# A fused attention and two-layer MLP kernel: gated values written where the sums read them, new orders on all engines

## The chip, the cores and the metric

One core of one Trainium2 chip. The metric is the device time of one execution in microseconds (us). The kernel has five instruction streams, each with its own order: TensorE (PE; its weight loads are shown as PEld), VectorE (DVE), ScalarE (ACT), GpSimd (POOL) and SyncE (SP), which here issues every DMA. Streams meet only at semaphores. Times of rows are us from the start of the span of one profiled execution.

## The reference

Attention over 4 x 8 heads of 576 tokens (a mean-pooled softmax attention, repeated to full length, plus a local one) gives x of 2304 x 512. Then two layers, all in fp32:

```
gate = 1 / (1 + exp(-(x @ w_gate)));  val = x @ w_val        # w_gate, w_val: 512 x 1536
x = (gate * val) @ w_out                                     # 1536 x 512
h = x @ w_in                                                 # 512 x 2048
g = h * (1 / (1 + exp(-1.702 * h)))
out = g @ w_out                                              # 2048 x 512
```

## The kernel before

**Precision.** A product of two fp32 matrices is made of three matmuls in the format fp32r: every operand is split into a rounded part (hi, a CAST on ACT) and the rest (lo, a subtraction on DVE or POOL); hi*hi, hi*lo and lo*hi are added in PSUM.

**Strassen's scheme.** Every product of layers 1 and 2 into the hidden dimension is a block of 2 x 2 quarters made of seven products p1 to p7 instead of eight. A product is six matmuls of 128 x 384 (two halves of the depth, three matmuls each). It needs sums of quarters of the weights (S1 to S4, made once, stored in DRAM as `w_split` and fetched for each block) and of x (T1 to T4, made once for each pass over 768 tokens; there are three passes for each layer). A block has three PSUM banks: x gets p1, then p6, p7 and p4 on top; y gets p2; z gets p5 and p3. ACT copies x out three times (`snap_p1`, `snap_u2`, `snap_u3`, lines 1069 to 1084); p6 waits for the first copy, p7 for the second, p4 for the third. DVE adds the copies to the other banks (`c11` line 1585, `c22` line 1595, `c12` line 1599); the four quarters of a result are called 11, 21, 12 and 22. p3 waits for `c22`, since z is read by it.

**Groups and pairs.** A group is 256 columns of the hidden dimension. In layer 1 it has two blocks (gate and value: 14 products), in layer 2 one (7). Groups 0 to 5 (layer 1, first pass) are multiplied by w_out in the plain way (`from_one_to_one`, `second`). Groups 6 to 41 are taken in pairs, and the output product of a pair is in Strassen's form too: `second_pair` (lines 776 to 778), seven tiles of two column blocks, six matmuls each, so 14 steps of one product's length. There are six pairs of layer 1 (`pair_of_one`, c = 6 to 16) and twelve of layer 2 (`pair_of_two`, c = 18 to 38, and `last_pair`). For c, the second group of the pair is d = c + 1, and n = c + 2 opens the next pair. The stages of a pair: PE runs p4 and p3 of c's last block, the blocks of d, all but p4 and p3 of n's first block, then the 14 steps.

**What the output product needs.** From the gated values: hi (`hi11`, ..., line 1150) and lo (`low11`, ..., line 1608) of quarters 11, 21 and 22, and of four sums T1 = g12 - g11, T3 = g22 - g12, T2 = T3 + g11, T4 = g21 - T2 (`make_t1`, ... lines 1644 to 1665 on DVE, `hi_t` line 1167 on ACT, `low_t` line 1669 on DVE). Gated values lie in the PSUM banks, written in place by `gate` (DVE, layer 1) or `gelu` (ACT, line 1109). Since T1 and T3 overwrite banks, ACT copies 11, 21 and 12 to SBUF first (`save11`, `save21`, `save12`, lines 1131, 1138, 1144), into a free part of the buffer `g_f`. From w_out (c's pair of groups): SP's `load_pair` (line 390) loads two blocks of 512 KB into `raw`; ACT rounds (`v_a12`, `v_a11`, `v_a22` line 1028 from `raw`; `v_s1` to `v_s4` line 1035 from sums); POOL makes the four sums (`pair_sum`, line 2036) and seven lo parts (`pair_low`, line 2040) in `split_pair`. The sum VS3 is made last, when the sixth tile of the pair before has been read. `load_pair(c + 2)` waits for all seven lo parts of c.

**Other work.** Eight jobs (`job_a`, `job_s` on ACT, `job_sums`, `job_lows` on POOL) split the weights of layer 2 during layer 1. Before each pass T1 to T4 of x are made (`next_t2_sums`, `next_t1_t3_sums`, `next_t4_sums` on POOL, lines 2074 to 2133), rounded on ACT (line 999), and their lo parts made on POOL (line 2067).

**What sets the order.** Every stream's order is written out by hand: `pair_of_one`, `pair_of_two` and `last_pair` exist once for ACT and once for DVE, `step` and `head` for PE, the loops at the end of the sync and gpsimd blocks for the rest. Each engine does its list in order, so an instruction that waits holds all behind it.

## Time and profile before

| what | us |
|---|---|
| median of 3 runs (lowest, highest) | 1040.64 (1037.27, 1041.56) |
| the profiled execution | 1044.47 |
| its span | 1042.8 |
| PE busy in it | 915.2 |
| PEld, DVE, ACT, POOL busy | 871.8, 585.1, 528.3, 594.9 |

The rows further below are lines of the profile. A group row of instructions reads: line, engine, operation, output<-inputs, shapes, count | busy us, mean ns of one | idle time before them and what ended it. "X <- Y" in a list of waits means that X started when Y had ended. Matmuls overlap, so that a busy time of PE counts more than the time between starts: the starts of two matmuls are what to read.

### The profile page before, as it was taken

Reading aid. Unit: us, or ns where it says so; the run is one execution under the profiler, and the core shown is the slowest. Engines: PE = TensorE matmul, PEld = TensorE weight load, DVE = VectorE, ACT = ScalarE, POOL = GpSimd, SP = SyncE. Lnnn points to the kernel's source line nnn. Section 1 sums busy time; section 2 is a strip of 40 time slices with the busy share of each in tenths; the row PEclk is TensorE's granted clock in tenths of the full one; section 3 lists DMA queues with packets and bytes.
Section 4 is the critical chain, followed back from the end, with each engine's and each line's share of the span. In section 5 each row is a group of like instructions: output and inputs, shape, how many; then the busy total and the mean of one; then the engine's idle time right before and its main releaser. Section 6 shows DMA issues by size and latency. Waiting matters only on the chain.

```text
span 1042.8 us, 18514 instructions
## 1 busy us (share of the span) xinstructions
PE 915.2 (88%) x6638; PEld 871.8 (84%) x6638; DVE 585.1 (56%) x1128; ACT 528.3 (51%) x1191; POOL 594.9 (57%) x483
## 2 busy tenths in 40 slices
PE   9999999997969898799898788888788888798798
PEld 7787999997868898798898788878788878788787
DVE  6677454453545555375555466555466555465476
ACT  5787645543445354355444545534545534534552
POOL 5688898897167375727365653444663444631531
PEclk9999999998989999999999999898999988898899
DMA  8775566875465946284936245335236425236321
GB/s 319 246 215 199 207 221 244 331 295 180 152 233 170 353 122 222 77 303 154 361 116 211 70 133 162 91 112 161 70 133 222 125 78 162 66 120 190 108 72 61
DMA packets 74778, 184.27 MB, mean 177 GB/s; under 512 B 5568, under 2 KB 31168, under 8 KB 71872
## 3 DMA queue, kind: packets, MB, share of 16 engines
q1 hardware_dynamic: 74688, 183.10, 51.4%
q8 instruction: 53, 0.87, 0.4%
q14 instruction: 37, 0.30, 0.1%
HBM read 141.66 MB, written 41.42 MB: 176 GB/s over the span
## 4 chain that ended last, share of the span: by engine, by line
PE 52%; POOL 19%; issue 10%; ACT 8%; DMA 6%; DVE 4%; SPq 1%; ACTq 0%; DVEq 0%; POOLq 0%
POOL v L2040 7%; PE o_ps L776 5%; POOL v_f L2036 5%; PE o_ps L778 5%; PE o_ps L777 5%; PE d_ps L632 4%; POOL xs_lo L2067 4%; DMA raw<-in_w_out_dram 4%; PE d_ps L633 4%; PE d_ps L634 4%; PE o_ps L623 4%; PE s_ps L632 3%; PE s_ps L634 3%; PE s_ps L633 3%; DMA job_raw<-in_w_in_dram 2%
## 5 line engine op out<-in xcount | busy, mean ns | idle before, releaser
L2040 POOL TENSOR_TENSOR v<-raw,v 128x512 fp32r<-128x512 f32 x54 | 69.3, 1283 | 247.8 <-ACT v L1028 234.2
L776 PE MATMUL o_ps<-g_hi,v 128*128 128x384 f32 x504 | 177.4, 352 | 29.8 <-DVE att L1713 29.8
L632 PE MATMUL d_ps<-xs_hi,w 128*128 128x384 f32 x360 | 128.6, 357 | 68.8 <-ACT snap L1072 44.2
L778 PE MATMUL o_ps<-g_hi,v 128*128 128x384 f32 x504 | 175.5, 348 | 0.0
L777 PE MATMUL o_ps<-g_lo,v 128*128 128x384 f32 x504 | 175.4, 348 | 0.0
L1713 DVE TENSOR_TENSOR att<-o_ps,att 128x384 f32<-128x384 f32 x212 | 117.2, 556 | 73.8 <-PE o_ps L778 72.2
L632 PEld LDWEIGHTS d_ps<-xs_hi,w 128*128 128x128 f32 x360 | 71.1, 197 | 79.2 <-ACT snap L1072 49.6
L776 PEld LDWEIGHTS o_ps<-g_hi,v 128*128 128x128 f32 x504 | 100.1, 199 | 34.6 <-POOL v L2040 18.7
L634 PE MATMUL d_ps<-xs_hi,w 128*128 128x384 f32 x360 | 125.2, 348 | 0.0
L633 PE MATMUL d_ps<-xs_lo,w 128*128 128x384 f32 x360 | 125.1, 348 | 0.0
L632 PE MATMUL s_ps<-xs_hi,w 128*128 128x384 f32 x300 | 106.0, 353 | 19.6 <-ACT snap L1078 9.4
L634 PE MATMUL s_ps<-xs_hi,w 128*128 128x384 f32 x300 | 104.3, 348 | 0.0
L633 PE MATMUL s_ps<-xs_lo,w 128*128 128x384 f32 x300 | 103.9, 346 | 0.0
L2040 POOL TENSOR_TENSOR v<-v_f,v 128x512 fp32r<-128x512 f32 x72 | 91.1, 1280 | 21.2 <-ACT v L1035 21.2
L777 PEld LDWEIGHTS o_ps<-g_lo,v 128*128 128x128 f32 x504 | 100.1, 199 | 0.0
L778 PEld LDWEIGHTS o_ps<-g_hi,v 128*128 128x128 f32 x504 | 99.5, 197 | 0.0
L1035 ACT CAST v<-v_f 128x512 fp32r<-128x512 f32 x72 | 43.2, 620 | 107.8 <-POOL v_f L2036 107.4
L632 PEld LDWEIGHTS s_ps<-xs_hi,w 128*128 128x128 f32 x300 | 59.0, 197 | 24.8 <-ACT snap L1078 11.3
L1167 ACT CAST g_hi<-t_ps 128x384 fp32r<-128x384 f32 x96 | 45.7, 483 | 66.4 <-DVE t_ps L1658 35.3
L2067 POOL TENSOR_TENSOR xs_lo<-xs_sum,xs_hi 128x768 fp32r<-128x768 f32 x24 | 43.8, 1830 | 57.7 <-ACT xs_hi L999 57.7
L1669 DVE TENSOR_TENSOR g_lo<-t_ps,g_hi 128x384 fp32r<-128x384 f32 x96 | 53.1, 553 | 34.4 <-ACT g_hi L1167 32.5
L633 PEld LDWEIGHTS d_ps<-xs_lo,w 128*128 128x128 f32 x360 | 71.2, 198 | 0.0
(173 smaller groups left out, 2182.0 us busy)
## 6 DMA issues: line engine op xcount, KB each, us to landing
w<-w_split SPq DMA_DIRECT2D x48, 768.0 KB, 5.3
w<-w_split SPq DMA_DIRECT2D x48, 512.0 KB, 5.1
w<-w_split SPq DMA_DIRECT2D x96, 256.0 KB, 3.4
w_split<-w SPq DMA_DIRECT2D x12, 1792.0 KB, 6.7
raw<-in_w_out_dram SPq DMA_DIRECT2D x36, 512.0 KB, 6.2
w_split<-job_w SPq DMA_DIRECT2D x8, 1792.0 KB, 9.7
vw<-in_v_win_dram SPq DMA_DIRECT2D x16, 390.0 KB, 4.9
raw<-in_w_gate_val_dram SPq DMA_DIRECT2D x12, 512.0 KB, 4.0
```

Source lines behind the costliest of these rows:

```text
L632: pe.matmul(bank, wh[:, cols], xh[:, c, :], start=(start and c == 0), stop=False, skip_group_check=True)
L633: pe.matmul(bank, wh[:, cols], xl[:, c, :], start=False, stop=False, skip_group_check=True)
L634: mm = pe.matmul(bank, wl[:, cols], xh[:, c, :], start=False, stop=(c == 1), skip_group_check=True)
L776: pe.matmul(bank, vh, gh, start=(start and k == c), stop=False, skip_group_check=True)
L777: pe.matmul(bank, vh, gl, start=False, stop=False, skip_group_check=True)
L778: mm = pe.matmul(bank, vl, gh, start=False, stop=(k == c + 1), skip_group_check=True)
L1167: nc.scalar.copy(g_hi[k % 2][:, t, :], bank[LAST[k] % 2]).then_inc(thi_ready[t], 1)
L1669: vec.tensor_tensor(g_lo[k % 2][:, t, :], bank[LAST[k] % 2], g_hi[k % 2][:, t, :], ALU.subtract).then_inc(t_ready[t], 1)
L1713: vec.tensor_tensor(part, value, part, ALU.add).then_inc(y_added, 1)
L2036: gp.tensor_tensor(v_f[:, :, 1, v_part, :], a, c, op).then_inc(vp_summed, 1)
L2040: gp.tensor_tensor(v_all[:, :, 1, v_part, :], source, v_all[:, :, 0, v_part, :], ALU.subtract).then_inc(vp_ready, 1)
L2067: gp.tensor_tensor(xs_lo[at][:, :, :], source, xs_hi[at][:, :, :], ALU.subtract).then_inc(x_ready, 1)
```

## The change

Per part, in the order of the diff:

- The buffer. `gelu` and `gate` write quarters 11, 12 and 21 of the groups from 6 on straight to where the saves put them (`gated_at`), and wait for that part of `g_f` to be free (`SLOT`, `g_free`). The saves are gone. `round_g`, `low`, `make_t1`, `make_t3` read from there. Quarter 22 stays in its bank.
- Waits on PE and DVE. `free_x` and `c22` wait for `gated` where they waited for `g_ready`.
- PE. In `step` p3 of the block before stands ahead of p2. In group 5 three steps of the output product stand ahead of p4.
- ACT. The casts of w_out's parts are spread: VA12 and VA11 of the next pair at the end of a pair, VS1, VS2, VS4 behind the next pair's first `snap_p1`, VS3 and VA22 behind its `snap_u3`; in the pairs beside a change of pass (`late`) later still. For pair 6 the first two casts move into group 5. Jobs and roundings of x are spread out as well.
- DVE. The sums T1 and T3 of x for passes 1 to 5 (`x_t1`, `x_t3`), and T2 of pass 1 (`x_t2`), are made by DVE; the order of the lows, sums and additions is changed.
- POOL. VS3's sum comes before the lo parts of VS2 and VS4; these, VS3's and VA22's lo part form `split_pair_end`. In layer 2 this comes after the next pass's T1 and T3 lo parts.
- SP. In layer 2 `load_pair` is issued two fetches earlier; the loads of jobs 4 and 7 one block later.

The core of the diff, with its indentation shortened:

```diff
-V_HIS = {VA12: 1, VS1: 2, VA11: 3, VS2: 4, VS4: 5, VS3: 6, VA22: 7}
+V_HIS = {VA12: 1, VA11: 2, VS1: 3, VS2: 4, VS4: 5, VS3: 6, VA22: 7}
+SLOT = {11: T2, 12: T2, 21: T4}
...
@@ buffers of the gated values
+def gated_at(k, n, bank):
+if k < G1 or n == 22:
+    return bank[LAST[k] % 2]
+return (saved_11_at if n == 11 else saved_12_at if n == 12 else saved_21_at)(k)
 def count(b, n):
...
@@ sync
             load_pair(c + 2)
-        if c in (G1 + 2, G1 + 8) and b == FIRST[c + 1]:
+        if c in (G1 + 2, G1 + 8) and b == LAST[c + 1]:
             store_job(3 if c == G1 + 2 else 6)
...
-        fetch_3(b + 1)
-        fetch_12(b + 2)
+    fetch_3(FIRST[c + 2])
     load_pair(c + 2)
+    fetch_12(FIRST[c + 3])
+    fetch_3(FIRST[c + 3])
+    fetch_12(FIRST[c + 3] + 1)
     for q in (3, 4):
         if c == START[q + 1] + 2:
             store(q)
...
@@ tensor: free_x, step
+        elif k < G1:
+            pe.wait_ge(g_ready[21], k + 1)
         else:
-            pe.wait_ge(g_ready[21], k + 1)
+            pe.wait_ge(gated[21], k + 1)
...
+    p3(b - 1)
     p2(b)
-    p3(b - 1)
     p6(b)
     p5(b)
     p7(b)
...
@@ tensor: from_one_to_one
-    p4(n)
-    second(k, 3)
-    p3(n)
-    second(k, 4)
-    p1(m)
-    second(k, 5)
+    if k == 5:
+        second(k, 3)
+        second(k, 4)
+        second(k, 5)
+        p4(n)
+        p3(n)
+        p1(m)
...
@@ scalar: gelu (save11, save21, save12 and their calls are taken out)
-    nc.scalar.activation(bank[FIRST[k] % 2], bank[FIRST[k] % 2], ACT.Gelu_apprx_sigmoid).then_inc(gated[n], 1)
+    if n in SLOT and (n != 21 or k < NG - 2) and (n != 11 or k != NG - 2):
+        act.wait_ge(y_ready, g_free(k, SLOT[n]))
+    nc.scalar.activation(gated_at(k, n, bank), bank[FIRST[k] % 2], ACT.Gelu_apprx_sigmoid).then_inc(gated[n], 1)
...
 def hi11(k):
     round_g(k, 11, y_bank)
...
@@ scalar: from_one_to_one
     snap_p1(n)
+    hi22(k)
+    hi21(k)
+    if k == 5:
+        round_t1(1)
+    sig11(k + 1)
     if k == 5:
         round_t3(1)
-    hi22(k)
-    hi21(k)
-    sig11(k + 1)
     snap_u2(n)
...
+    if k == 5:
+        v_a12(G1)
+        v_a11(G1)
 def pair_of_one(c):
...
@@ scalar: pair_of_one, the first half
         hi11(c)
         snap_u3(LAST[c])
+        v_s3(c)
+        v_a22(c)
     snap_p1(FIRST[d])
+    hi22(c)
+    hi21(c)
     if last:
         round_b11(q + 1)
-        round_b21(q + 1)
-    hi22(c)
-    save21(c)
-    hi21(c)
+    snap_u2(FIRST[d])
+    hi_t1(c)
     sig11(d)
+    if c == G1:
+        v_s1(c)
+    snap_u3(FIRST[d])
+    hi_t3(c)
     if c in (G1 + 2, G1 + 6, G1 + 8):
         job_a({2: 3, 6: 5, 8: 6}[c - G1])
-        job_s({2: 3, 6: 5, 8: 6}[c - G1])
-    snap_u2(FIRST[d])
-    save12(c)
-    hi_t1(c)
-    snap_u3(FIRST[d])
-    hi_t3(c)
     snap_p1(LAST[d])
     hi_t2(c)
+    if last:
+        round_b21(q + 1)
     sig22(d)
     sig21(d)
     hi_t4(c)
-    if c == G1:
-        v_a12(c)
-        v_s1(c)
-        v_a11(c)
-    snap_u2(LAST[d])
-    sig12(d)
     if c == G1:
         v_s2(c)
         v_s4(c)
         v_s3(c)
         v_a22(c)
-    save11(d)
+    if c in (G1 + 2, G1 + 6, G1 + 8):
+        job_s({2: 3, 6: 5, 8: 6}[c - G1])
+    if last:
+        round_t2(q + 1)
+    snap_u2(LAST[d])
+    sig12(d)
     hi11(d)
+    if c == G1:
+        job_a(2)
     snap_u3(LAST[d])
     if last:
-        round_t2(q + 1)
+        round_t1(q + 1)
     snap_p1(FIRST[n])
...
@@ scalar: pair_of_two
-    save12(c)
+    if not (first and q > 3):
+        v_s1(c)
+    if not late:
+        v_s2(c)
+        v_s4(c)
     gelu11(d)
     snap_u2(FIRST[d])
     hi_t1(c)
     hi_t3(c)
-    save11(d)
     hi11(d)
     snap_u3(FIRST[d])
-    v_a22(c)
+    hi_t2(c)
     if last:
         round_t1(q + 1)
+    elif late:
+        v_s1(c)
+    else:
+        v_s3(c)
+        v_a22(c)
     snap_p1(FIRST[n])
-    gelu22(d)
-    hi_t2(c)
-    gelu21(d)
-    save21(d)
-    hi21(d)
     hi_t4(c)
-    hi22(d)
     if last:
         round_t3(q + 1)
+    gelu22(d)
+    gelu21(d)
+    if last:
+        snap_u2(FIRST[n])
+    hi21(d)
     gelu12(d)
-    snap_u2(FIRST[n])
-    save12(d)
+    if not last:
+        snap_u2(FIRST[n])
+    hi22(d)
     hi_t1(d)
     snap_u3(FIRST[n])
+    if late:
+        v_s2(c)
+        v_s4(c)
     hi_t3(d)
+    if late:
+        v_s3(c)
+        v_a22(c)
+    hi_t2(d)
+    if not late:
+        v_a12(n)
+    if c == START[q] + 2 and q + 1 < len(PHASES):
+        round_t2(q + 1)
+    hi_t4(d)
     if first and q + 1 < len(PHASES):
         round_b11(q + 1)
         round_b21(q + 1)
-    hi_t2(d)
-    if c == START[q] + 2 and q + 1 < len(PHASES):
-        round_t2(q + 1)
-    v_a12(n)
-    hi_t4(d)
     gelu11(n)
     if last:
         round_t4(q + 1)
         round_b22(q + 1)
-    v_s1(n)
+    if late:
+        v_a12(n)
     v_a11(n)
-    save11(n)
     hi11(n)
     gelu22(n)
     hi22(n)
-    v_s2(n)
...
@@ vector: c22, gate, low, make_t1, sums of x
+        dve.wait_ge(g_ready[11], k + 1)
     else:
-        dve.wait_ge(g_ready[11], k + 1)
+        dve.wait_ge(gated[11], k + 1)
...
+    if k >= G1 and n in SLOT:
+        dve.wait_ge(y_ready, g_free(k, SLOT[n]))
+    vec.tensor_tensor(gated_at(k, n, bank), g_f[k % 2][:, 0, PIECE[n], :], bank[LAST[k] % 2], ALU.mult).then_inc(gated[n], 1)
...
     dve.wait_ge(ghi_ready[n], k + 1)
-    vec.tensor_tensor(g_lo[k % 2][:, PIECE[n], :], bank[LAST[k] % 2], g_hi[k % 2][:, PIECE[n], :], ALU.subtract
+    vec.tensor_tensor(g_lo[k % 2][:, PIECE[n], :], gated_at(k, n, bank), g_hi[k % 2][:, PIECE[n], :], ALU.subtract
                       ).then_inc(g_ready[n], 1)
...
-    dve.wait_ge(saved_12, strassen(k))
-    dve.wait_ge(ghi_ready[11], k + 1)
-    vec.tensor_tensor(z, z, saved_11_at(k), ALU.subtract).then_inc(t_made[T1], 1)
+    dve.wait_ge(gated[12], k + 1)
+    dve.wait_ge(gated[11], k + 1)
+    vec.tensor_tensor(z_bank[LAST[k] % 2], saved_12_at(k), saved_11_at(k), ALU.subtract).then_inc(t_made[T1], 1)
...
+def x_t1(q):
+    quarter = parts(PHASES[q][1])
+    wait_last(q, 1)
+    vec.tensor_tensor(xs_sum[ring(q, T1)][:, :, :], quarter[0, 1], quarter[0, 0], ALU.subtract).then_inc(xsum_ready[T1], 1)
+def x_t3(q):
+    quarter = parts(PHASES[q][1])
+    wait_last(q, 2)
+    vec.tensor_tensor(xs_sum[ring(q, T3)][:, :, :], quarter[1, 1], quarter[0, 1], ALU.subtract).then_inc(xsum_ready[T3], 1)
...
@@ vector: pair_of_one, its first half
     gate21(c)
-    low22(c)
-    c11(FIRST[d])
-    low21(c)
     c12(LAST[c])
     gate12(c)
+    low22(c)
     make_t1(c)
+    c11(FIRST[d])
     make_t3(c)
+    low21(c)
     low_t1(c)
     c22(FIRST[d])
     make_t2(c)
     low_t3(c)
     low_t2(c)
     make_t4(c)
+    low_t4(c)
     c11(LAST[d])
-    low_t4(c)
     c12(FIRST[d])
...
@@ vector: pair_of_two, its end
     low_t4(c)
     low21(d)
+    make_t1(d)
     low22(d)
-    make_t1(d)
+    low_t1(d)
+    add(c, 0)
     make_t3(d)
-    low_t1(d)
-    c11(FIRST[n])
-    add(c, 0)
     add(c, 1)
     make_t2(d)
     add(c, 2)
+    c11(FIRST[n])
+    add(c, 3)
     low_t3(d)
-    add(c, 3)
+    add(c, 4)
     low_t2(d)
-    add(c, 4)
+    add(c, 5)
     make_t4(d)
-    add(c, 5)
+    add(c, 6)
     low_t4(d)
-    for o in range(6, 10):
+    for o in range(7, 10):
         add(c, o)
     if n + 2 < NG:
         add(c, 10)
+        add(c, 11)
     low11(n)
-    if n + 2 < NG:
-        add(c, 11)
     c22(FIRST[n])
     if n + 2 < NG:
...
@@ gpsimd: split_pair and its new end; the loop of layer 2
     pair_low(c, VS1, v_f[:, :, 1, VS1, :])
+    pool.wait_ge(y_ready, v_free(c, VS3))
+    pair_sum(VS3, raw[:, :, V11, :], raw[:, :, V21, :], ALU.subtract)
+def split_pair_end(c):
+    steps = 4 * pair(c)
     pool.wait_ge(vp_summed, steps + 3)
     pair_low(c, VS2, v_f[:, :, 1, VS2, :])
     pair_low(c, VS4, v_f[:, :, 1, VS4, :])
-    pool.wait_ge(y_ready, v_free(c, VS3))
-    pair_sum(VS3, raw[:, :, V11, :], raw[:, :, V21, :], ALU.subtract)
     pair_low(c, VS3, v_f[:, :, 1, VS3, :])
     pair_low(c, VA22, raw[:, :, V22, :])
...
+        if last:
+            next_t1(q + 1)
+            next_t3(q + 1)
+        split_pair_end(c)
         if q + 1 < len(PHASES):
             if c == START[q]:
                 next_b11(q + 1)
...
-                late_x(q + 1)
+        if last:
+            next_t4_sums(q + 1)
+            next_t4(q + 1)
+            next_b22(q + 1)
         if c + 2 < NG:
             split_pair(c + 2)
```

## Rows read from the trace of the kernel before

**Rows 1.** The page: busy time of PE, DVE, ACT and POOL.
```profile
PE 915.2 (88%) x6638; PEld 871.8 (84%) x6638; DVE 585.1 (56%) x1128; ACT 528.3 (51%) x1191; POOL 594.9 (57%) x483
```
**Rows 2.** Stretches: start:end, length, busy (x) of PE, PEld, DVE, ACT, POOL; PEclk, DMA share, GB/s.
```profile
150.00:200.00 50.00, 50.00 (x290) 50.00 (x289) 25.57 (x48) 26.44 (x45) 44.04 (x37) 1.00 0.74 273
240.90:268.60 27.70, 22.35 (x110) 21.48 (x109) 9.86 (x19) 9.87 (x19) 13.01 (x8) 0.88 0.37 117
268.60:586.10 317.50, 272.69 (x1473) 264.48 (x1472) 175.50 (x333) 149.84 (x310) 179.93 (x135) 0.95 0.58 200
586.10:1006.00 419.90, 355.40 (x1825) 344.30 (x1824) 236.66 (x456) 209.73 (x460) 195.83 (x144) 0.92 0.40 129
1006.00:1042.80 36.80, 29.66 (x164) 27.80 (x162) 23.72 (x46) 15.00 (x34) 10.35 (x9) 1.00 0.12 43
```
**Rows 3.** Waits of PE: who waited for whom, us in total, times, longest.
```profile
PE d_ps L632 <- ACT snap L1072: 44.2, 17, 5.8
PE o_ps L776 <- DVE att L1713: 29.8, 14, 4.1
```
**Rows 4.** Timeline, head of the pair c = 38: start, us, what [idle before <- releaser].
```profile
979.10 1.28 POOL L2036 TENSOR_TENSOR v_f<-raw 128x512 f32<-128x512 f32 x1
...
980.41 0.62 ACT L1035 CAST v<-v_f 128x512 fp32r<-128x512 f32 x1 [3.43 <-POOL v_f L2036]
980.94 0.47 ACT L1109 ACTIVATE s_ps<-s_ps 128x384 f32<-128x384 f32 x1
...
983.14 0.69 PE L632 MATMUL d_ps<-xs_hi,w 128*128 128x384 f32 x1 [3.04 <-ACT snap L1072]
```
**Rows 5.** Timeline, the output product of the pair c = 36.
```profile
956.44 0.33 PE L776 MATMUL o_ps<-g_hi,v 128*128 128x384 f32 x1
...
957.20 1.07 SPq L390 DMA_DIRECT2D raw<-in_w_out_dram  x2
...
957.48 0.33 PE L776 MATMUL o_ps<-g_hi,v 128*128 128x384 f32 x1
...
965.66 0.62 ACT L1028 CAST v<-raw 128x512 fp32r<-128x512 f32 x1 [5.40 <-DMA raw<-in_w_out_dram]
966.19 0.47 ACT L1167 CAST g_hi<-t_ps 128x384 fp32r<-128x384 f32 x1
...
966.69 0.56 DVE L1669 TENSOR_TENSOR g_lo<-t_ps,g_hi 128x384 fp32r<-128x384 f32 x1 [3.19 <-ACT g_hi L1167]
...
967.86 0.41 PE L776 MATMUL o_ps<-g_hi,v 128*128 128x384 f32 x1 [2.87 <-DVE att L1713]
```
**Rows 6.** Timeline, the first pair of layer 1, c = 6.
```profile
288.07 3.69 POOL L2040 TENSOR_TENSOR v<-v_f,v 128x512 fp32r<-128x512 f32 x3
...
293.02 0.62 ACT L1035 CAST v<-v_f 128x512 fp32r<-128x512 f32 x1 [4.26 <-POOL v_f L2036]
...
295.43 0.66 PE L632 MATMUL d_ps<-xs_hi,w 128*128 128x384 f32 x1 [8.48 <-ACT snap L1084]
295.89 0.52 PE L633 MATMUL d_ps<-xs_lo,w 128*128 128x384 f32 x1
```
**Rows 7.** Timeline, job 4 in the pair c = 8, and a head in layer 1.
```profile
350.19 0.83 ACT L1062 CAST job_w<-job_raw 128x768 fp32r<-128x768 f32 x1 [3.03 <-DMA job_raw<-in_w_in_dram]
...
354.63 0.45 PE L632 MATMUL s_ps<-xs_hi,w 128*128 128x384 f32 x1 [4.80 <-ACT snap L1078]
...
377.92 0.45 PE L632 MATMUL d_ps<-xs_hi,w 128*128 128x384 f32 x1 [1.60 <-ACT snap L1072]
378.21 0.34 PE L633 MATMUL d_ps<-xs_lo,w 128*128 128x384 f32 x1
```
**Rows 8.** Groups of instructions: a sum of x on POOL, a save, a lo part on DVE.
```profile
L2074 POOL TENSOR_TENSOR xs_sum<-att 128x768 f32<-128x768 f32 x6 | 11.0, 1838 | 0.0
L1138 ACT COPY g_f<-d_ps 128x384 f32<-128x384 f32 x23 | 11.1, 481 | 6.1 <-DVE d_ps L1604 5.8
L1608 DVE TENSOR_TENSOR g_lo<-t_ps,g_hi 128x384 fp32r<-128x384 f32 x66 | 36.4, 552 | 44.2 <-ACT g_hi L1150 44.2
```

## Prediction before the run

> **What bounds the kernel now.** The page's busy times come first [rows 1]: PE 915.2 us of 1042.8, no other engine over 57%. So PE, or what holds it. How much PE needs is read where nothing holds it: 290 matmuls in 50.00 us at clock 1.00 [rows 2], 0.172 us each, and 1.04 us from one output step to the next [rows 5]. A product and a step are both six matmuls: 1.04 us. Before 240.9 us (attention, first pass) PE hardly stops. Behind it come 594 of them: 18 in the rest of group 5, 245 in layer 1's six pairs, 304 in the eleven full pairs of layer 2, 27 in the end. Against the stretches [rows 2]:
>
> - 240.9 to 268.6: 18.7 us of work, 9.0 lost
> - 268.6 to 586.1: 254.8 of work, 62.7 lost, 10.4 a pair
> - 586.1 to 1006.0: 316.2 of work, 103.7 lost, 9.4 a pair
> - to the end: 28.1 of work, 8.7 lost, 3.1 of it the last addition and store
>
> In all 617.8 of work and 184.1 lost, at clocks of 0.88 to 0.95 in the first three. The list of waits says to whom [rows 3]: 17 waits for `snap_p1` (44.2 us) and 14 for an addition by DVE (29.8). Each is one chain.
>
> First chain [rows 4]: POOL makes VS3's sum at 979.10, which must wait for the tile before; ACT stands 3.43 us at `v_s3` for it, with `gelu21`, `save21`, `hi21`, `gelu12` and `snap_p1` behind; p6 starts at 983.14 after 3.04 us. It recurs at the head of every pair; in layer 1 it costs 1.60 [rows 7].
>
> Second [rows 5]: `load_pair` is issued at 957.20, its data are cast at 965.66, and ACT stands 5.40 us at `v_a12` with `hi_t4` behind it. DVE's `low_t4` waits 3.19 with the additions behind it, and PE 2.87 for a bank.
>
> Third, once each: the whole chain of the first pair (8.48 us, [rows 6]), and job 4's and job 7's loads, waited for by ACT in front of a snap (4.80 us, [rows 7]).
>
> Then the clock. Behind the stop of 8.48 us the second matmul follows the first after 0.46 us and takes 0.52 (the 1.2 GHz level); behind one of 1.60 us it follows after 0.29 and takes 0.34 (2.4 GHz) [rows 6, 7]. The longer stops are paid again as slow work.
>
> **The change, part by part.** I walk a steady pair of layer 2 with t = 0 at p4(c), products at multiples of 1.04, readers 0.2 behind an end; ACT needs 0.4 us from start to start for 384 columns and 0.53 for 512 [rows 5], DVE 0.5 [rows 5, 8], POOL 1.28 [rows 4].
>
> The saves: nine groups of instructions, 108 copies of 0.48 us [rows 8], 52 us of ACT. Six a pair, 2.4 us of ACT's time; ACT is half idle (528.3 busy, [rows 1]), so alone they are worth only what stands in front of a snap: `save21`, 0.5 a head.
>
> First chain. `snap_p1(d)` now has `gelu21` (1.2), `hi21` (1.7) and `gelu12` (2.9) in front and starts when p1(d) has ended, 3.3; p6(d) is due at 4.2. Wait gone. Next late is `snap_u2(d)`: behind it came `v_s1`, `v_s2`, `v_s4` and `gelu11(d)`, so 5.7 to 6.15, with p7(d) due at 6.24. It holds if VS4's sum is there, which POOL ends at 30 of the pair before, 0.9 of this one. `v_s3` stands at 8.3; POOL makes its sum at 5.6 to 6.9. Hidden.
>
> p3(d), moved ahead of p2, is due at 9.36. `c22(d)` ends about 9.0 on DVE, behind `low11(d)`: 0.3 of slack. The p2 that it passes needs `low_t3(c)`, done at 8.1; p5(n), due at 12.5, needs `low_t4(c)`, which ends at 11.6.
>
> Second chain. SP passes `load_pair` over two fetches, but it still waits for VA22's lo part, now POOL's last, at 12; four 1.28 us instructions stand behind each other there. So it is issued at 12, against about 13.7 now (end of p7(n), free of stops), and the fetches follow it, not in front. With the 8.5 us of now [rows 5] the cast can start at 20.5, and sooner with nothing queued in front. `hi_t4(d)` is wanted at 22.1, since `make_t4(d)` ends there. Wait gone, slack 1.1. The weights held behind the load are for the pair after, from 31.2 on. `gelu11(n)` gets a wait for the tenth step, 25.2, with `v_a11`, `hi11` behind it; the save waited for the same, and `low11(n)` is now behind the addition that PE needs. No cost.
>
> Pairs of layer 1: the same by 43.7 us. `snap_p1` loses `v_s3` from its front; the jobs' casts stand behind snaps or, for 4 and 7, behind `hi_t4(d)`, when the step that PE needs is made. The load of job 4 comes 7 us later, and POOL's sums of the next pair with it, at 45 to 48, which `v_s4` at 48 just meets. The first pair's casts of VA12 and VA11 go into group 5, so VS3 is made some 10 us before it is asked for.
>
> Sums of x: POOL loses five T1 and T3, 1.84 each [rows 8], and DVE gains ten. DVE's price for 768 columns is not in the trace: between 0.55 (a row of 384, [rows 8]) and 1.84 (POOL's). I take 1.0, twice the pace of 384. In the last pair of a pass that puts T3's lo part at 13.7 with p7(n) due at 13.5. In the four `late` pairs VA22's lo part ends at 21, raw data come at 28.5, `hi11(n)` stands behind their cast, and p3(n) waits about 1.
>
> New losses, then: group 5 2.2 (x's lo parts of T1, T4 and B22, still one behind another on POOL, come 1.1, 0.3 and 0.8 after PE wants them); layer 1 4.8 (0.8 a pair, a guess from the slack of its walk); layer 2 9.6 (four late pairs 1.5 each, three with x's parts queued on POOL 0.8, four others 0.3); the end 6.1 (3.1 as now, and 3.0 of its stops). Sum 22.7, against 184.1: 240.9 + 617.8 + 22.7 = 881.4.
>
> Low parts of 11 and 21 and `make_t1` now read two operands in SBUF, six a pair; every DVE row before has one in PSUM. Beside busy POOL their price lies between 0 (a row of 0.55, [rows 8]) and 1.28 each if one waits out a POOL instruction. `make_t1(c)` and `low11(d)` fall into POOL's run from 4.4 to 12; 0.3 of it is slack. I take 0.45 us a pair, nearest to the low end, for 17 pairs: 8. And five places a pair with 0.3 us of slack or less: between 0 and 1.5 a pair; I take 0.5, 9 in all. 898.4, and 1.7 outside the span: 900.1 beside 1044.47. The median of the runs is 0.4% under the profiled execution: 896.8, **897 us**.
>
> The page "SBUF — State Buffer" of the Trainium skill, under "Who interferes with whom", says that a VectorE instruction with two SBUF inputs and a GpSimd instruction that reads SBUF exclude each other for a whole instruction, and that the order of issue decides. No row before shows such a pair of instructions. By it the 8 us above would be 8 to 45.
>
> **The rivals.**
>
> *Every hold on the shared way to SBUF reaches PE.* Two-operand reads wait out POOL instructions: 6 x 1.28 = 7.7 us a pair, a third of it beyond slack, 2.5 a pair in 18 pairs: 45 in place of 8, 934. For it: POOL runs back to back where `make_t1(c)` stands. Against: only `c22(d)` and p3(d) are near. This is the page's rule at its dearest.
>
> *The load stays last.* VA22's lo part slips, `v_a12` is waited for as now: the 29.8 us for additions [rows 3] stay, and a third as much for the clock: 897 + 40 = 937. For it: the order on SP hardly gains two us. Against: 1.1 us of slack, and no fetch in front.
>
> *Slower.* POOL keeps the way to SBUF through a run of instructions back to back (three in 3.69 us, [rows 6]). A pair has a run of 7.6 us where `make_t1(c)` is due and one of 3.8 at `low11(n)`: 11.4 less 1.7 of slack, 9.7, and 3 of slow clock: 12.7 in 18 pairs, 881 + 229 = 1110. It turns slower from (1042.8 - 881.4) / 18 = 9.0 us a pair. Against: POOL's instructions wait for ACT in between.
>
> *It doesn't do what it says.* Had another engine been the last releaser, `v_s3`'s wait would move to another cast in front of a snap: 3.04 us a pair as now, within 0.5% of 1040.6.
>
> **How the numbers follow.** Forecast 0.67 (its own range 875 to 925), holds 0.12, load 0.12, slower 0.05, no effect 0.04. What a measurement here can tell from no change is about 0.5%. Faster 0.67 + 0.12 + 0.12 = 0.91, same 0.04, slower 0.05. The range runs from 872 (no holds, no small slack missed, and half of the new losses of the pairs: 874 + 1.7, less 0.4%) to 958 (either of the two middle cases with its price a half over).
>
> **What would show it.** PE's waits for `snap_p1` fall from 44.2 us to under 8, those for additions from 29.8 to under 6; PEclk in layer 2 at 0.98 or more; W's casts from `raw` stand under 1 us for their DMA; no ACT copy into the buffer from a bank; POOL's 1.28 us rows keep their length. Wrong it is if `low11` or `make_t1` show starts delayed to POOL's ends, if PE stops at p3 for `c22`, or if `v_a12` still waits for its DMA.

## The result, and the profile after

The kernel after takes 888.14 us (median of 4 runs, 887.71 to 891.31); the kernel before 1041.1 (4 runs, 1037.27 to 1043.6). The ratio is 0.854, 95% interval 0.8507 to 0.8573. The forecast was 897, the range 872 to 958. The profiled execution took 887.71 us with a span of 886.0.

The page of the kernel after, engines' busy time and the granted clock in 40 slices, beside [rows 1]:
```profile
PE 863.6 (97%) x6638; PEld 830.4 (94%) x6638; DVE 639.4 (72%) x1140; ACT 486.2 (55%) x1083; POOL 591.5 (67%) x471
...
PEclk9999999999999999999999999999999999999999
```
PE issues the same 6638 matmuls and is busy 51.6 us less: that is mostly the clock (the last section counts the slow work). ACT lost 108 instructions and 42 us. DVE is busy 54 us longer with only twelve instructions more, x's sums, which take 18 us. The rest is the surprise of this case: DVE instructions that last longer than before. It is taken up under a_pool_short.

The same four stretches, beside [rows 2] (start:end, length, busy of PE, PEld, DVE, ACT, POOL, PEclk, DMA share, GB/s):
```profile
238.40:259.40 21.00, 19.72 (x109) 18.52 (x109) 9.98 (x20) 7.23 (x14) 10.96 (x6) 1.00 0.54 175
259.40:523.90 264.50, 259.38 (x1472) 254.87 (x1471) 194.45 (x336) 133.24 (x269) 174.94 (x128) 1.00 0.69 240
523.90:849.40 325.50, 321.42 (x1826) 316.35 (x1825) 265.35 (x462) 186.75 (x399) 202.97 (x143) 1.00 0.48 166
849.40:886.00 36.60, 29.46 (x164) 27.86 (x162) 26.23 (x46) 12.89 (x28) 11.12 (x9) 1.00 0.12 43
```
27.7 became 21.0, 317.5 became 264.5, 419.9 became 325.5, and the end kept its length (36.8 and 36.6). Less the work of 18.7, 254.8, 316.2 and 28.1, what is lost is 2.3, 9.7, 9.3 and 8.5: 29.8 in place of 184.1. The granted clock is 1.00 in each of the four.

What PE waits for, beside [rows 3]:
```profile
PE d_ps L642 <- DVE s_ps L1610: 3.4, 4, 1.4
PE o_ps L788 <- DVE att L1752: 2.7, 2, 2.3
PE o_ps L788 <- issue: 2.5, 2, 1.2
PE s_ps L642 <- POOL xs_lo L2129: 2.3, 4, 0.8
...
PE d_ps L642 <- ACT snap L1098: 0.8, 2, 0.6
```
`snap_p1` is gone from the list (44.2 us before), additions are at 2.7 (29.8 before). First now stands L1610, `c22`. (In this kernel L1092, L1098 and L1104 are the three copies `snap_p1`, `snap_u2`, `snap_u3`.)

The pair c = 36, the one whose output product is in [rows 5]; its t = 0 is 824.09:
```profile
827.41 0.48 ACT L1092 COPY snap<-d_ps 128x384 f32<-128x384 f32 x1
...
829.73 0.48 ACT L1098 COPY snap<-d_ps 128x384 f32<-128x384 f32 x1
...
832.94 0.55 DVE L1610 TENSOR_TENSOR t_ps<-snap,t_ps 128x384 f32<-128x384 f32 x1
...
833.64 0.41 PE L642 MATMUL t_ps<-xs_hi,w 128*128 128x384 f32 x1
...
836.70 0.81 SPq L399 DMA_DIRECT2D raw<-in_w_out_dram  x2
...
842.80 0.62 ACT L1048 CAST v<-raw 128x512 fp32r<-128x512 f32 x1
...
846.49 0.48 ACT L1170 CAST g_hi<-t_ps 128x384 fp32r<-128x384 f32 x1 [3.06 <-DVE t_ps L1680]
```
`snap_p1` at 3.3, `snap_u2` at 5.6, `load_pair` at 12.6, the cast of its data at 18.7 with no wait for the DMA, `hi_t4(d)` at 22.4 behind DVE's `make_t4`. (In the whole trace one such cast still waits for its DMA, 1.4 us.) The tight spot is `c22(d)`, ended at 9.4, and p3(d) at 9.55 where 9.36 was due.

### The profile page after: what moved, and what is told of

Its sections match the earlier page's. It is cut to its first block, busy times and chain, and to the rows that moved or that the text cites. A ratio compares the mean times of both kernels' runs of the same rounds, so it can differ in the third digit from the quotient of the medians.

```text
span 886.0 us, 18369 instructions
## 1 busy us (share of the span) xinstructions
PE 863.6 (97%) x6638; PEld 830.4 (94%) x6638; DVE 639.4 (72%) x1140; ACT 486.2 (55%) x1083; POOL 591.5 (67%) x471
## 4 chain that ended last, share of the span: by engine, by line
PE 81%; issue 6%; DVE 5%; POOL 4%; ACT 2%; DMA 1%; SPq 1%; DVEq 0%; ACTq 0%; POOLq 0%
PE o_ps L788 9%; PE o_ps L790 9%; PE o_ps L789 9%; PE d_ps L642 6%; PE o_ps L633 6%; PE d_ps L644 5%; PE d_ps L643 5%; PE s_ps L642 5%; PE s_ps L644 5%; PE s_ps L643 5%; PE t_ps L642 3%; PE t_ps L644 3%; PE t_ps L643 3%; PE o_ps L606 1%; POOL v L2099 1%
## 5 line engine op out<-in xcount | busy, mean ns | idle before, releaser
L788 PE MATMUL o_ps<-g_hi,v 128*128 128x384 f32 x504 | 169.7, 337 | 5.4 <-DVE att L1752 2.7
L790 PE MATMUL o_ps<-g_hi,v 128*128 128x384 f32 x504 | 169.6, 337 | 0.0
L789 PE MATMUL o_ps<-g_lo,v 128*128 128x384 f32 x504 | 169.4, 336 | 0.0
L2099 POOL TENSOR_TENSOR v<-v_f,v 128x512 fp32r<-128x512 f32 x72 | 95.3, 1343 | 51.4 <-ACT v L1055 51.4
L642 PE MATMUL d_ps<-xs_hi,w 128*128 128x384 f32 x360 | 122.3, 340 | 5.9 <-DVE s_ps L1610 3.4
L644 PE MATMUL d_ps<-xs_hi,w 128*128 128x384 f32 x360 | 120.7, 335 | 0.0
L643 PE MATMUL d_ps<-xs_lo,w 128*128 128x384 f32 x360 | 120.6, 335 | 0.0
L642 PE MATMUL s_ps<-xs_hi,w 128*128 128x384 f32 x300 | 101.9, 340 | 2.8 <-POOL xs_lo L2129 2.3
L788 PEld LDWEIGHTS o_ps<-g_hi,v 128*128 128x128 f32 x504 | 94.7, 188 | 7.2 <-issue 4.2
L644 PE MATMUL s_ps<-xs_hi,w 128*128 128x384 f32 x300 | 100.5, 335 | 0.0
L789 PEld LDWEIGHTS o_ps<-g_lo,v 128*128 128x128 f32 x504 | 94.8, 188 | 0.0
L790 PEld LDWEIGHTS o_ps<-g_hi,v 128*128 128x128 f32 x504 | 94.7, 188 | 0.0
L642 PEld LDWEIGHTS d_ps<-xs_hi,w 128*128 128x128 f32 x360 | 67.6, 188 | 11.0 <-issue 7.3
L1624 DVE TENSOR_TENSOR g_lo<-g_f,g_hi 128x384 fp32r<-128x384 f32 x69 | 63.1, 914 | 17.6 <-ACT g_hi L1153 17.6
L2129 POOL TENSOR_TENSOR xs_lo<-xs_sum,xs_hi 128x768 fp32r<-128x768 f32 x24 | 44.8, 1870 | 42.5 <-ACT xs_hi L1019 42.5
L644 PEld LDWEIGHTS d_ps<-xs_hi,w 128*128 128x128 f32 x360 | 67.6, 188 | 0.0
```

The lines of the kernel that those rows point to most:

```text
L642: pe.matmul(bank, wh[:, cols], xh[:, c, :], start=(start and c == 0), stop=False, skip_group_check=True)
L643: pe.matmul(bank, wh[:, cols], xl[:, c, :], start=False, stop=False, skip_group_check=True)
L644: mm = pe.matmul(bank, wl[:, cols], xh[:, c, :], start=False, stop=(c == 1), skip_group_check=True)
L788: pe.matmul(bank, vh, gh, start=(start and k == c), stop=False, skip_group_check=True)
L789: pe.matmul(bank, vh, gl, start=False, stop=False, skip_group_check=True)
L790: mm = pe.matmul(bank, vl, gh, start=False, stop=(k == c + 1), skip_group_check=True)
```

## The experiments

How long the four stretches (the same matmuls, counted from the end) last in each profiled execution:
```
                  group 5  layer 1  layer 2   end   median of runs
before              25.9    317.5    420.0   36.8       1041.1
b_s3_moved          24.4    306.3    374.7   36.8        985.0
b_load_first        23.1    319.2    399.5   36.8       1017.5
b_both              24.1    307.8    349.3   36.7        960.4
after               21.0    264.5    325.5   36.6        888.1
a_saves_back        21.0    270.8    325.9   35.8        893.9
a_load_last         21.1    266.0    339.8   37.1        904.7
a_first_back        21.0    275.2    325.5   36.6        901.2
a_jobs_back         21.0    280.5    325.5   36.5        904.5
a_turns_back        21.0    264.7    341.7   37.2        905.0
a_xsums_pool        22.5    264.9    324.9   37.0        889.8
a_p3_late           21.0    271.7    326.9   36.5        898.2
a_pool_short        21.0    266.2    322.5   34.1        883.8
n_low_behind        21.0    263.2    324.5   34.7        884.9
```
Group 5 is counted here from its first matmul, which in the kernel before starts at 242.7, so that the stop of 1.6 us in front of it is left out. The kernel after and its nine variants start it anywhere from 238.2 to 241.2: that is scatter of the part in front, so small differences are read from the stretches. Each stretch is that of one profiled execution.

**b_s3_moved: the first chain alone, on the kernel before.**
```diff
                 snap_u3(FIRST[d])
+                v_s3(c)
                 v_a22(c)
...
                 v_s4(n)
-                if n + 2 < NG:
-                    v_s3(n)
```


> The kernel before with one thing of the change: ACT's cast of VS3's sum stands ahead of VA22's cast in the next pair, no longer in front of snap_p1. Theory (two chains, each with its own share of the slow clock): the stops for snap_p1 at the heads, some 33 us in layer 2 and 8 in layer 1, go; jobs' stop of 5.8 stays; at 0.4 us of slow matmuls for each us of stop (49.6 beside 124.8 in the trace of before) 38 + 15 = 53 us less: 988, range 980 to 1000. Rival 'the wait moves on' (VS4's cast or snap_u2 becomes late by as much): 1030 to 1041. Rival 'ACT's time counts' (the saves, which stay here): 1041.

Measured 985.04 us, ratio 0.9447 (0.937 to 0.9523): 56 us less than the 1041.1 of the kernel before, 53 expected. 11 of them come in layer 1 and 45 in layer 2. Both rivals fall; the wait for VS3's sum in front of `snap_p1` was the releaser.

**b_load_first: the second chain alone.**
```diff
-                for b in (FIRST[c + 1], FIRST[c + 2]):
-                    fetch_3(b + 1)
-                    fetch_12(b + 2)
+                fetch_3(FIRST[c + 2])
                 load_pair(c + 2)
+                fetch_12(FIRST[c + 3])
+                fetch_3(FIRST[c + 3])
+                fetch_12(FIRST[c + 3] + 1)
```


> The kernel before with one thing of the change: in layer 2 SyncE issues the weight pair's load ahead of two fetches. Theory: the additions' stops in layer 2, some 27 us, go with 11 of slow clock: 1003, range 995 to 1012; VA12's cast waits under 1 us for its DMA. Rival 'load stays last' (it waits for VA22's lo part all the same and gains under 1 us): 1035 to 1041.

Measured 1017.54 us, ratio 0.9753 (0.9667 to 0.9838). 24 us, 20.5 of them in layer 2, where 38 were expected: both the theory's range and the rival's are missed. The casts no longer wait for the load at all, and the waits for additions fell from 29.8 to 13.4 us. What stays are three long ones (3.5 to 4.1 us), in the output product at each change of pass, and those of the end. The three have another cause, a chain that the theory didn't see: GpSimd makes x's lo parts ahead of the pair's sums, and ACT stands at `v_s1`, with `hi11` and DVE's additions behind it:
```profile
725.92 0.62 ACT L1036 CAST v<-v_f 128x512 fp32r<-128x512 f32 x1 [5.51 <-POOL v_f L2037]
```

**b_both.**

> The kernel before with both of these edits. Theory (the chains are apart): the savings add up, 53 + 38 = 91 us: 950, range 938 to 965. What is left to the kernel after (888) are the first pair's 8.5 us, the jobs' 9.6, the ends of passes and their clock. Rival 'one loop' (the second chain takes up what the first leaves): about 985, no better than the better of the two alone.

Measured 960.4 us, ratio 0.9213 (0.9152 to 0.9274): 81 us (91 expected, within the range), where the two alone give 56 and 24. The chains are apart, and "one loop" falls. But 72 us lie between this kernel and the one after. The first three stretches of it:
```profile
241.30:265.50 24.20, 22.03 (x109) 21.48 (x110) 10.02 (x19) 8.58 (x17) 11.22 (x7) 0.86 0.39 118
265.50:573.20 307.70, 272.87 (x1471) 265.35 (x1471) 175.28 (x333) 149.97 (x310) 180.24 (x134) 0.95 0.60 206
573.20:922.60 349.40, 332.77 (x1826) 327.15 (x1826) 236.64 (x456) 209.70 (x460) 196.65 (x144) 0.96 0.45 155
```
Layer 1 holds 43 of the 72 and still runs at 0.95: single long stops, each paid again in part as slow matmuls. The next seven kernels undo one part of the change each.

**a_saves_back: in-place writing undone, all orders kept.**
```diff
-            if k < G1 or n == 22:
+            if True:
                 return bank[LAST[k] % 2]
...
             def hi21(k):
+                if k >= G1:
+                    save21(k)
...
-                        pe.wait_ge(gated[21], k + 1)
+                        pe.wait_ge(g_ready[21], k + 1)
```


> The kernel after with the in-place writing undone alone: GELU and gate write their bank again, 108 copies of 0.48 us bring the values into the buffers on ACT, low parts and make_t1 read a bank; all new orders stay. Theory: the copies stand beside PE's work but for 0.3 to 0.5 us a head, and no DVE instruction of groups reads two operands in SBUF any more, so L1624's low parts are back at 0.55 us: 892, range 885 to 900. Rival 'ACT's time is what counts': 888 + 40 to 52 = 928 to 940. Rival 'holds are dear': below 880.

Measured 893.92 us, ratio 0.858 (0.8519 to 0.864; it overlaps the one of after, so the difference rests on the stretches). "ACT's time is what counts" falls: 108 copies are back and cost 5.8 us, all of it in layer 1 (6.3 by the stretches). The theory's size is right and its place is wrong. The waits of PE, first row, and what DVE does ahead of one of them (at 314.84):
```profile
PE d_ps L643 <- DVE g_lo L1644: 5.7, 6, 0.9
...
312.75 0.57 DVE L1679 TENSOR_TENSOR t_ps<-t_ps,g_f 128x384 f32<-128x384 f32 x1 [1.35 <-ACT g_f L1161]
...
314.15 0.55 DVE L1644 TENSOR_TENSOR g_lo<-d_ps,g_hi 128x384 fp32r<-128x384 f32 x1
```
Six pairs, 0.9 us each: PE's next p1 needs the bank of piece 21, which with the old writing is free only when its low part is made; written in place, when it is gated. That low part is late itself, for `make_t1` in front of it on DVE waits 1.35 us for ACT's copy `save12` (L1161). So one reader more and one copy in the chain act together, and no run parts them; ACT's busy time is not what counts. In layer 2 the bank is free in time either way (325.9 beside 325.5).

**a_load_last.** The diff of b_load_first turned round, on the kernel after.

> The kernel after with one thing undone: in layer 2 SyncE issues the weight pair's load behind the two fetches again. Theory: the raw data come too late for the cast ahead of hi_t4 and the additions' stops come back, 7 pairs of 2 to 3 us and 3 passes' ends of about 4 with 0.4 us of slow clock for each: 25 to 45 us more, 920, range 908 to 935. Rival 'the new order on ACT is enough' (in the late pairs VA12's cast stands far back, and the wait for it has slack in the others): under 895.

Measured 904.7 us, ratio 0.8639 (0.8597 to 0.8681): 16.6 us, 14.3 of them in layer 2. It lies between the two, below the theory's range and above the rival's. The chain is back; where it is longest, ACT's cast, then PE:
```profile
704.36 0.62 ACT L1047 CAST v<-raw 128x512 fp32r<-128x512 f32 x1 [5.50 <-DMA raw<-in_w_out_dram]
...
707.20 0.69 PE L787 MATMUL o_ps<-g_hi,v 128*128 128x384 f32 x1 [2.71 <-DVE att L1751]
```
At the other output products PE loses 1.1 to 2.2 us, with 0 to 1.8 us of slow matmuls behind.

**a_first_back.**
```diff
-                if k == 5:
-                    v_a12(G1)
-                    v_a11(G1)
...
                 hi_t4(c)
                 if c == G1:
+                    v_a12(c)
+                    v_a11(c)
+                    v_s1(c)
                     v_s2(c)
```


> The kernel after with one thing undone: the first pair's casts of VA12 and VA11 are made in the pair's own first half (behind hi_t4) and not in group 5. Theory: the stop of 8.5 us in front of the second step comes back, with 3 us of slow matmuls behind it (3.13 with both edits on the kernel before): 899, range 896 to 903. Rival: POOL's sums, not the casts, bind the first pair: under 892.

Measured 901.23 us, ratio 0.8612 (0.8563 to 0.866), 13 us by the medians, as expected, and 10.7 in the profiled execution (898.59 us), all in layer 1: the stop of [rows 6] is back unchanged,
```profile
281.80 0.69 PE L642 MATMUL d_ps<-xs_hi,w 128*128 128x384 f32 x1 [8.49 <-ACT snap L1098]
```
and 2.1 us of slow matmuls follow it. The other 2.4 us of the medians aren't in this trace.

**a_jobs_back.**
```diff
-                    if c in (G1 + 2, G1 + 8) and b == LAST[c + 1]:
+                    if c in (G1 + 2, G1 + 8) and b == FIRST[c + 1]:
...
                 sig11(d)
+                if c in (G1 + 2, G1 + 6, G1 + 8):
+                    job_a({2: 3, 6: 5, 8: 6}[c - G1])
+                    job_s({2: 3, 6: 5, 8: 6}[c - G1])
...
                 hi21(d)
+                if c in (G1, G1 + 2, G1 + 8):
+                    job_a({0: 2, 2: 4, 8: 7}[c - G1])
+                    job_s({0: 2, 2: 4, 8: 7}[c - G1])
                 snap_u2(FIRST[n])
```


> The kernel after with one thing undone: the casts of the jobs (weights that are split and stored again during layer 1) stand where they stood before, in front of snap_u2, and the loads of jobs 4 and 7 are issued one step earlier again. Theory: the stops of 5.8 and 4.85 us in front of p7, with 2.6 and 3.3 of slow matmuls behind them, come back: 905, range 900 to 910. Rival: the earlier load hides half of it: 896.

Measured 904.48 us, ratio 0.8653 (0.8598 to 0.8707), 16.3 us, all in layer 1, as expected. Job 4, beside [rows 7]:
```profile
328.63 0.83 ACT L1082 CAST job_w<-job_raw 128x768 fp32r<-128x768 f32 x1 [3.35 <-DMA job_raw<-in_w_in_dram]
...
331.59 1.05 ACT L1086 CAST job_w<-job_f 128x1024 fp32r<-128x1024 f32 x1 [2.13 <-POOL job_f L2077]
...
333.07 0.69 PE L642 MATMUL s_ps<-xs_hi,w 128*128 128x384 f32 x1 [4.77 <-ACT snap L1098]
```

**a_turns_back.**
```diff
-                late = last or first and q > 3
+                late = False
...
+                v_s3(c)
+                v_a22(c)
                 if last:
                     round_t1(q + 1)
...
-                    if last:
-                        next_t1(q + 1)
-                        next_t3(q + 1)
                     split_pair_end(c)
...
+                        next_t1(q + 1)
+                        next_t3(q + 1)
                         next_t4_sums(q + 1)
```


> The kernel after with one thing undone: at the two turns of a pass inside layer 2 the casts of the pair's weights keep their ordinary places on ACT and GpSimd makes the pair's four last lo parts before those of T1 and T3 (the sums of T1 and T3 stay on DVE). Theory: PE stops again for x's lo parts at a turn; with both edits on the kernel before a turn cost 7.4 (three stops) and 6.3 to 7.5 us (one stop for an addition, where after has none); of the first kind all comes back, of the second little: 888 + 2 x 7 = 902, range 896 to 912. Rival 'x's sums on DVE are enough': under 892.

Measured 905.0 us, ratio 0.8658 (0.8609 to 0.8708): 16.9 us, 8 for each turn (the change from one pass to the next), nearly all in layer 2, as expected. PE's waits, the first two rows:
```profile
PE d_ps L642 <- ACT snap L1098: 6.1, 3, 2.9
PE d_ps L642 <- POOL xs_lo L2126: 4.5, 2, 2.2
```

**a_xsums_pool.**
```diff
+            def pool_sums(q):
+                b = LAST[START[q] - 1]
+                pool.wait_ge(in_done[b % 2], count(b, 1))
+                sum_t1(q)
+                pool.wait_ge(in_done[b % 2], count(b, 2))
+                sum_t3(q)
...
+                        pool_sums(q + 1)
                         next_t1(q + 1)
```


> The kernel after with one thing undone: T1's and T3's sums of x are made by GpSimd again in front of T1's lo part (q = 1 to 5), no DVE instruction takes them. Theory: on POOL they put 2 x 1.84 us in front of the lo parts that the first products of a pass wait for; five turns of a pass lose 3.6 us and 1.8 of slow clock each: 915, range 905 to 925. Rival 'the place of the order is what helped, not the engine': within 3 us of 888.

Measured 889.79 us, ratio 0.8496 (0.8455 to 0.8537). The expectation misses: which engine makes these sums is worth 1.5 us at the first turn and nothing at the other four. The rival (within 3 us of 888) came true. With the casts of the pair's weights moved behind them, x's parts have POOL's time; the place in the order is what counted, as a_turns_back shows for two of the turns.

**a_p3_late.**
```diff
                 p4(b - 1)
-                p3(b - 1)
                 p2(b)
+                p3(b - 1)
```


> The kernel after with one thing undone: in a step p3 of the block before stands behind p2 again. Theory (slack on both sides, as the stops of after leave it): c22, for which p3 waits, gets a step of 1.04 us more, so its stops of 0.6 to 1.1 us in a layer 1 pair and behind the turns go (2 to 3 us in all), and c12, gelu12 or gate12 and make_t1 behind it come 1.04 us later, of which their chains have more than that: 886, range 883 to 892. Rival 'the move of p3 was needed' (make_t1's chain is the one that sets the first output step or the bank of p5): each of 17 pairs loses 0.5 to 1 us and more: 897 to 905.

Measured 898.2 us, ratio 0.8613 (0.8551 to 0.8675): 10 us, the rival; the theory missed its range, and `c22`'s stops stay (3.0 of 3.4 us). By the stretches 7.2 us lie in layer 1 and 1.4 in layer 2. PE's waits, the first two rows:
```profile
PE o_ps L788 <- issue: 6.1, 6, 2.1
PE t_ps L642 <- DVE g_lo L1684: 3.3, 6, 1.2
```
p3 one product earlier starts `c12`, the gate and T1, T3, T2, T4 behind it. With p3 late again, p5 of the next block waits for the bank of T4 (second row), and the first output step of four pairs of layer 1 starts 0.7 to 2.3 us late (in the first row, where the kernel after has two waits, 2.5 us). In layer 1, where gates stand between, that chain has no slack left.

Six of the seven parts undone (the load stands in b_both too) add up to 60 of the 70 us that the stretches of b_both and the kernel after differ by. The other 10 are not tested one by one.

**a_pool_short: what the length of GpSimd's instructions does.**
```diff
-                gp.tensor_tensor(v_f[:, :, 1, v_part, :], a, c, op).then_inc(vp_summed, 1)
+                gp.tensor_tensor(v_f[:, :, 1, v_part, 0:8], a[:, :, 0:8], c[:, :, 0:8], op).then_inc(vp_summed, 1)
...
-                gp.tensor_tensor(v_all[:, :, 1, v_part, :], source, v_all[:, :, 0, v_part, :], ALU.subtract).then_inc(vp_ready, 1)
+                gp.tensor_tensor(v_all[:, :, 1, v_part, 0:8], source[:, :, 0:8], v_all[:, :, 0, v_part, 0:8], ALU.subtract).then_inc(vp_ready, 1)
```


> The kernel after with GpSimd's sums and lo parts of layer 2's and layer 1's output weights cut from 256 to 8 columns of each of the two halves (same count, order and waits); left out are the lo parts of these weights in the products (the hi parts are read in their place, the same number of matmuls) and ACT casts from the raw weights. Theory (holds): a DVE instruction with both operands in SBUF waits for the GpSimd instruction under way; with short ones g_lo from the buffer falls from 914 ns mean to under 620, make_t1 from 939 to 1282 to under 620, and the rows of x, where GpSimd still has 1.84 us instructions, stay above 700; c22's stops (3.4 us) go: 880 to 886. Rival 'own price' (two operands in SBUF take 0.74 us or more by themselves): the rows keep their means, time within 2 us of 888.

First the groups of the kernel after (partitions x elements, count, busy us, mean ns, idle before); L1624 are the low parts of gated values, L1659 is `make_t1`, L2095 the sums of w_out's parts:
```profile
L1624 DVE TENSOR_TENSOR g_lo<-g_f,g_hi 128x384 fp32r<-128x384 f32 x69 | 63.1, 914 | 17.6 <-ACT g_hi L1153 17.6
L1659 DVE TENSOR_TENSOR t_ps<-g_f 128x384 f32<-128x384 f32 x24 | 22.5, 939 | 0.0
L1659 DVE TENSOR_TENSOR d_ps<-g_f 128x384 f32<-128x384 f32 x11 | 14.1, 1282 | 0.0
...
L2095 POOL TENSOR_TENSOR v_f<-raw 128x512 f32<-128x512 f32 x36 | 50.0, 1390 | 4.0 <-PE o_ps L790 4.0
```
then the first three in a_pool_short,
```profile
L1624 DVE TENSOR_TENSOR g_lo<-g_f,g_hi 128x384 fp32r<-128x384 f32 x69 | 48.1, 697 | 15.6 <-ACT g_hi L1153 15.6
L1659 DVE TENSOR_TENSOR t_ps<-g_f 128x384 f32<-128x384 f32 x24 | 18.2, 757 | 0.0
L1659 DVE TENSOR_TENSOR d_ps<-g_f 128x384 f32<-128x384 f32 x11 | 6.2, 560 | 0.0
```
and the same low parts in a_saves_back, where one operand comes from a bank beside the full-length GpSimd work:
```profile
L1644 DVE TENSOR_TENSOR g_lo<-t_ps,g_hi 128x384 fp32r<-128x384 f32 x66 | 36.3, 550 | 16.7 <-ACT g_hi L1167 16.7
```
"Own price" falls: where no GpSimd instruction is under way, the two-operand form takes 560 ns. A DVE instruction that waits for GpSimd's in this way is called held. My bound of 620 is missed by two means (697 and 757). Of 108 rows 19 are still long, 13 of them in layer 1, each beside one of GpSimd's jobs or parts of x, which kept their length; I had charged the weights' instructions alone with the hold. The time is 883.83 us, ratio 0.8443 (0.8403 to 0.8483): 4.3 us faster, 3.0 in layer 2 and 2.5 at the end, and 1.7 slower in layer 1. The slower part is a hold as well: a job's lo part of 2.40 us catches the first pair's `make_t1`, which takes 2.38 us (0.81 in the kernel after), and the first output step behind it comes 1.4 us late, with 1.1 of slow matmuls:
```profile
279.02 2.38 DVE L1659 TENSOR_TENSOR t_ps<-g_f 128x384 f32<-128x384 f32 x1
...
282.89 0.41 PE L788 MATMUL o_ps<-g_hi,v 128*128 128x384 f32 x1 [1.27 <-issue]
```
So 4.3 us is what is left after such chances. The holds themselves fell from 44.8 to 14.9 us, and with short instructions GpSimd is also done sooner; the run can't tell the two apart.

**n_low_behind: the three held instructions behind what PE waits for.**
```diff
-                low11(n)
                 c22(FIRST[n])
                 if n + 2 < NG:
                     add(c, 12)
                     add(c, 13)
+                low11(n)
                 low22(n)
...
                 low_t2(c)
-                make_t1(d)
-                low21(d)
                 add(c - 2, 12)
-                low22(d)
+                low21(d)
                 add(c - 2, 13)
+                make_t1(d)
+                low22(d)
```


> The kernel after with three moves on DVE alone: low11(n) stands behind c22(n) and the last two additions instead of in front of them, and in the last pair low21(d) and make_t1(d) stand behind the additions of the steps before. Theory: an instruction with two operands in SBUF is held by GpSimd's instruction under way (1.93 us at 642.65, 1.27 at 850.10, 1.62 at 864.85 in the trace of after), and here it holds what PE waits for; behind c22 the hold costs nothing: stops of 1.0, 1.0, 1.5 and 1.8 of 2.5 us go, 883, range 880 to 886. Rival 'the hold moves with it' (low22 and the gate chain behind it become late by the same time): 886 to 890, stops of PE at p5 or p3 in their place.

The kernel after at a turn (DVE, POOL and PE by start):
```profile
642.32 1.85 POOL L2129 TENSOR_TENSOR xs_lo<-att,xs_hi 128x768 fp32r<-128x768 f32 x1
642.65 1.93 DVE L1624 TENSOR_TENSOR g_lo<-g_f,g_hi 128x384 fp32r<-128x384 f32 x1 [0.82 <-ACT g_hi L1153]
644.11 1.61 POOL L2099 TENSOR_TENSOR v<-raw,v 128x512 fp32r<-128x512 f32 x1
...
644.51 0.55 DVE L1610 TENSOR_TENSOR s_ps<-snap,d_ps 128x384 f32<-128x384 f32 x1
...
645.20 0.41 PE L642 MATMUL d_ps<-xs_hi,w 128*128 128x384 f32 x1 [0.84 <-DVE s_ps L1610]
```
and n_low_behind at the same place:
```profile
641.90 0.55 DVE L1610 TENSOR_TENSOR s_ps<-snap,d_ps 128x384 f32<-128x384 f32 x1
...
643.99 0.76 DVE L1624 TENSOR_TENSOR g_lo<-g_f,g_hi 128x384 fp32r<-128x384 f32 x1
...
644.44 0.41 PE L642 MATMUL d_ps<-xs_hi,w 128*128 128x384 f32 x1
```
Measured 884.85 us (881.62 to 887.73), ratio 0.8468 (0.8429 to 0.8507), the fastest version with the whole computation. Its median is 3.3 us under that of after; the stretches give 1.3, 1.0 and 1.9 us. The stops for `c22` of 1.0 and 1.0 us are gone and that of 1.5 is 0.3; at the last stop, for an addition, 1.9 of 2.5 us are left. The 1.3 us of layer 1 are not the moves' doing: in the trace of after `make_t1` at 488.17 happened to be held for 1.7 us, with 1.8 of stops and slow matmuls behind it, and here it wasn't. The same instruction is held in some traces of the variants and free in others, so a difference of under 2 us in layer 1 proves nothing.

## Why the prediction was right

Right way, and within its own range. By its steps, in the profiled execution, forecast 900.1 and measured 887.7:

- **The two chains.** `v_s3` in front of `snap_p1`, and `load_pair` in front of `hi_t4`: each shown alone, and they add up. The walk of the steady pair holds to within 0.5 us at most places: `snap_p1` 3.3 (3.3 forecast), `snap_u2` 5.6 (5.7 to 6.15), load 12.6 (12), cast 18.7 (20.5 at the latest), `hi_t4(d)` 22.4 (22.1), `c22(d)` 9.4 (9.0).
- **The single stops.** First pair 11 to 13 us, jobs 16 us, with their slow matmuls, as the prediction's third point had them. Pass turns are 17; in the forecast they were only a loss of 1.5 us for a late pair, not named among the gains.
- **The losses in all.** Forecast 39.7 us (22.7 of new losses, 8 for holds, 9 for small slacks), measured 29.8. Stops of PE behind a held DVE instruction, with the slow matmuls behind them, come to some 8.6 us in the trace of after: 1.8 behind `make_t1` at 488.17, 2.2 at three `c22` in layer 2 (563, 683, 804), 2.2 at the `c22` of the two turns there, 0.7 at 852.0 and 1.7 at 867.1 (the last two by what a_pool_short takes away). So the 8 us for the holds were about right. This sum is read from one trace; a_pool_short and n_low_behind, which each take away a part of it, give 4.3 and 3.3 us.
- **New losses.** Without the holds: group 5 2.3 us (2.2 forecast), layer 1 7.9 (4.8; "0.8 a pair, a guess"), layer 2 4.9 (9.6), the end 6.1 (6.1): 21.2 beside 22.7, partly by luck. Layer 1 was put too low, since each of its two turns of a pass costs 3 to 4 us (0.7 to 0.9 for xs_lo, 1.4 for the first output product, the rest slow), and layer 2 too high.
- **The term that was mis-sized** is the 9 us for five places a pair with little slack. No loss is left over for it. 9, and 1.5 for the new losses, less 0.6 for the holds, plus 2.5 us that the part in front of group 5 was shorter, which is scatter: 12.4, the difference.
- **The saves** were put at nothing "but what stands in front of a snap: `save21`, 0.5 a head". The size was about right (5.8 us), the mechanism not: PE waits in layer 1 for a bank that is read once more, by a low part that a copy delays. And p3's move, which I gave 0.3 us of slack and no gain, is worth 10.
- **x's sums on DVE.** 1.0 us was taken for 768 columns. Unheld it is 0.95 (the least of T1's); held, 1.5 to 2.4 (T3's five). Bounds of 0.55 to 1.84 were too narrow above, and it cost nothing.
- **"Every hold reaches PE"** (0.12) saw rightly that there are holds: 75 of the 108 low parts and T1s on two buffers are lengthened. But they are 44.8 us together, where its 7.7 a pair would make 138, and some 9 of them reach PE, not 45. "The load stays last" (0.12) falls, and at 16.6 us its price was less than half of the 40 given. "Slower" (0.05) needed POOL to keep the way through a run; the holds end with each instruction (below).

Of the marks that were to show it right, two fail: GpSimd's 1.28 us rows did not keep their length (means of 1.32 to 1.42), and one cast from `raw` waits 1.4 us for its DMA. Of those that were to show it wrong, one came true: PE does stop at p3 for `c22`, 3.4 us in all. None of `low11` and `make_t1` starts late; they last longer, a sign I had not named.

## What to carry to other kernels

Here ACT was half idle and still held up PE, since its instructions stood in the wrong order: find the one wait that stands in front of what the bound engine needs (twice here, 56 and 24 us), before taking work from the idle engine (108 copies: 6 us). The long stops of b_both (3.6 to 8.7 us) were each paid again in part, by 1.9 to 4.2 us of slow matmuls, so that single ones (first pair, jobs, turns of a pass: 44 us by the stretches) are worth as much as 2.6 us in each of 17 pairs. A DVE instruction that reads two buffers beside a busy GpSimd lasted up to 4.1 times as long (2.27 us for 0.55): keep it behind what PE waits for.

## What the runs showed of the hardware

A DVE `tensor_tensor` with both operands in SBUF, started while a GpSimd instruction was under way, lasted 0.55 us plus the rest of that instruction, less some 0.13 us. At 642.65 it started 1.52 us ahead of the end of POOL's and lasted 1.38 us too long; all 75 long rows fit this to 0.01 us, and beside none of the 33 short ones was a GpSimd instruction under way. Its start in the trace is on time; it is the row that grows. GpSimd waits in turn: its next instruction took 1.61 us, and the sums of L2095 took 1.39 us on average (1.28 in [rows 4]). So the two take turns, instruction by instruction, and a run of GpSimd instructions doesn't shut DVE out. The longest row of 384 columns, 2.27 us at 488.17, started 0.01 us ahead of a GpSimd instruction of 1.84 us and waited for the whole of that one. The Trainium skill, "SBUF — State Buffer", under "Who interferes with whom", says that a VectorE instruction with two SBUF inputs contends with a GpSimd instruction that reads SBUF, that the lock is exclusive, and that the order of issue decides who blocks: the trace agrees.

The clock: the granted clock rose from 0.88, 0.95 and 0.92 in the first three stretches to 1.00. Call a stop a matmul that starts over 0.5 us later than 0.17 us behind the one before, and slow work all that the others take beyond 0.17 us (small waits are in it). From group 5 on the kernel before has 124 us of stops and 55 of slow work, b_both 60 and 36, the kernel after 16 and 8.5. In b_both the stops of 3.6 to 8.7 us are followed by 1.9 to 4.2 us of slow work each; in the kernel after, where no stop is over 2.5 us, by 0.1 to 1.5. In the kernel before only 43 of the 124 us are stops of 3.6 us and more; most are of 1.4 to 3.4. Their length alone doesn't tell what follows: a stop of 3.2 us at 820.9 has 0.5 us of slow work behind it, one of 3.2 at 942.7 has 3.4. Together the change took away 109 us of stops and 46 of slow work, 153 us by the medians.
